# The layer norm's weight folded into the second matrix of the first MLP, on one core

## The reference, cut to what matters

```python
def _moe_ref(x, w_in, w_out, g_ln):          # x 2304 x 512, w_in 512 x 1024, w_out 1024 x 512
    h = x @ w_in
    h_max = np.max(h, axis=-1, keepdims=True)
    e = np.exp(h - h_max)
    sm = e / (np.sum(e, axis=-1, keepdims=True) + 1e-09)
    solu = h * sm
    mu = np.mean(solu, axis=-1, keepdims=True)
    var = np.mean((solu - mu) ** 2, axis=-1, keepdims=True)
    ln = (solu - mu) / np.sqrt(var + 1e-06) * g_ln
    return (ln @ w_out).astype(np.float32)
```

## Time and profile before

| | us |
|---|---|
| median of three runs | 934.86 (934.52 to 937.16) |
| the profiled execution, its own time | 934.9 |
| its span, first to last instruction | 933.2 |
| PE busy | 896.9 (96%) |
| DVE busy | 764.9 (82%) |
| ACT busy | 500.2 (54%) |
| POOL busy | 431.7 (46%) |

### The profile page before, as it was taken

The page is one execution under the profiler, slowest core; times in us unless marked ns, Lnnn a source line. Parts: engine busy times, 40 slices in busy tenths (PEclk is TensorE's granted clock), DMA queues, the critical chain, the costliest instruction groups (busy, mean ns, idle before and its releaser), DMA issues.

```text
span 933.2 us, 15150 instructions
## 1 busy us (share of the span) xinstructions
PE 896.9 (96%) x5416; PEld 740.5 (79%) x5416; DVE 764.9 (82%) x1306; ACT 500.2 (54%) x936; POOL 431.7 (46%) x445
## 2 busy tenths in 40 slices
PE   3899999999999999999999899999999999999997
PEld 1566666666667798998999788989999998989996
DVE  4889989899992948367362699999999999999997
ACT  2677777778773634334242555545545455545443
POOL 0443444444661833142140455656565556556563
PEclk9999999999999999999999999999999999999999
DMA  9234323403210100000000620000000000000000
GB/s 227 81 64 102 77 52 77 103 26 77 95 46 1 34 12 1 1 1 1 1 7 6 225 81 1 35 1 1 35 1 1 35 1 1 34 0 0 34 0 34
DMA packets 29026, 37.56 MB, mean 40 GB/s; under 512 B 3488, under 2 KB 16800, under 8 KB 28960
## 3 DMA queue, kind: packets, MB, share of 16 engines
q1 hardware_dynamic: 28240, 36.12, 14.0%
q10 hardware_dynamic: 720, 0.59, 0.3%
HBM read 31.98 MB, written 4.72 MB: 39 GB/s over the span
## 4 chain that ended last, share of the span: by engine, by line
DVE 49%; PE 44%; issue 4%; DMA 1%; ACT 1%; SPq 0%; POOL 0%; DVEq 0%
DVE g L835 13%; PE y_ps L1015 11%; PE s_ps L921 9%; PE o_ps L959 9%; PE t_ps L932 7%; DVE g_hi L839 7%; DVE g L825 7%; DVE g_lo L841 6%; PE h_ps L896 5%; DVE g L828 5%; DVE x_lo L691 2%; DVE solu L792 1%; DVE st_top L778 1%; DVE ln_lo L754 1%; DVE y_lo L767 1%
## 5 line engine op out<-in xcount | busy, mean ns | idle before, releaser
L433 POOL TENSOR_TENSOR w_lo<-w_raw,w_hi 128x512 fp32r<-128x512 f32 x96 | 131.8, 1373 | 161.3 <-ACT w_hi L613 161.3
L394 POOL TENSOR_SCALAR kept<-kept,inv 128x576 f32<-128x576 f32 x144 | 106.2, 755 | 155.6 <-DVE inv L728 155.6
L493 ACT ACTIVATE expd<-s_ps,ntop 128x576 f32<-128x576 f32 x144 | 104.8, 742 | 78.1 <-DVE ntop L696 78.1
L991 PE MATMUL m_ps<-y_hi,w_lo 128*128 128x384 f32 x384 | 130.9, 341 | 0.0
L991 PE MATMUL m_ps<-y_lo,w_hi 128*128 128x384 f32 x384 | 129.8, 338 | 0.0
L629 ACT ACTIVATE l<-u 128x384 f32<-128x384 f32 x96 | 50.6, 527 | 145.8 <-POOL u L441 145.8
L991 PE MATMUL m_ps<-y_hi,w_hi 128*128 128x384 f32 x384 | 128.5, 335 | 0.0
L441 POOL TENSOR_TENSOR u<-z,consts 128x384 f32<-128x384 f32 x96 | 105.9, 1103 | 41.9 <-ACT z L622 41.8
L696 DVE TENSOR_REDUCE ntop<-s_ps 128x1 f32<-128x576 f32 x144 | 106.1, 755 | 21.4 <-PE s_ps L921 15.1
L1072 PE MATMUL f_ps<-w_hi,g_hi 128*128 128x512 f32 x288 | 115.7, 402 | 8.1 <-DVE g_lo L841 8.1
L835 DVE TENSOR_TENSOR g<-g,l 128x384 f32<-128x384 f32 x96 | 119.1, 1240 | 2.8
(11 more groups left out here) (83 smaller groups left out, 1811.9 us busy)
## 6 DMA issues: line engine op xcount, KB each, us to landing
q_sb<-q_t SPq DMA_DIRECT2D x32, 288.0 KB, 5.2
v_sb<-v_main SPq DMA_DIRECT2D x16, 256.0 KB, 3.2
stage<-w_in SPq DMA_DIRECT2D x16, 256.0 KB, 2.7
w_raw<-w_out SPq DMA_DIRECT2D x8, 512.0 KB, 6.3
out<-o_sb SPq DMA_DIRECT2D x5, 768.0 KB, 3.5
k_sb<-k_t SPq DMA_DIRECT2D x21, 144.0 KB, 4.6
stage<-w_in SPq DMA_DIRECT2D x4, 512.0 KB, 10.1
stage<-w_out SPq DMA_DIRECT2D x4, 512.0 KB, 3.6
```

What stands on the lines that cost most here:

```text
L394: nc.gpsimd.tensor_scalar(kept[:, tile % RING, :], kept[:, tile % RING, :], inv[:, group % 2, k:k + 1], 1.0, ALU.mult, ALU.mult).then_inc( ...
L433: nc.gpsimd.tensor_tensor(w4[1][:, n % 2, :], w4_raw[:, n % F2, :], f32(w4[0][:, n % 2, :]), ALU.subtract).then_inc(w4lo_made, 1)
L991: last = nc.tensor.matmul(m_ps[n % 4][:, 0:GC], w[:, k, (n % F2) * P:(n % F2 + 1) * P], y[odd][:, k, :], start=(k == 0 and m == 0), stop=( ...
```

## The change

The weight g_ln is no longer multiplied into every row of ln. It is loaded with its 1024 values as a 128 x 8 tile (value k*128+p on partition p, column k), early on SP's queue. Since ln @ w_out sums over the hidden columns, the rows of w_out are scaled by it once: in `w_high` ScalarE multiplies each half (128 x 512) of a piece of w_out in place with an ACTIVATE whose scale is a column of that tile, waits for both, and then casts as before. This makes eight new instructions and four waits.

For each tile the product on VectorE (L807) goes. GpSimd makes ln = (solu + nmean) * rstd in one TENSOR_SCALAR with two pointer scalars in place of the TENSOR_TENSOR on ln (L421), straight from solu. The wait for the last transpose (lt_made) moves from VectorE to it. solu(t) on VectorE waits for ln(t-2), since GpSimd now reads the solu buffer. GpSimd's program of the first MLP is written out for all 18 tiles.

```diff
--- before.py
+++ after.py
@@ -99,6 +99,7 @@
         ident = sb("ident", [P, P])
         tau_sb = sb("tau_sb", [P, 1])
         consts = sb("consts", [P, 5])
+        gain = sb("gain", [P, F1])
 
         xt = sb("xt", [P, 2 * PG * C * GC])
 
@@ -139,12 +140,11 @@
         x_lo = sb("x_lo", [P, 2, C, P], FP32R, where=phase)
 
         ln = sb("ln", [P, 2, DFF1], where=phase)
-        gain = sb("gain", [P, DFF1], where=phase)
         e1 = sb("e1", [P, 2, DFF1], where=phase)
         solu = sb("solu", [P, 2, DFF1], where=phase)
         names = "top ntop esum esum_e inv ssum nmean sq msq var rstd"
         st = {n: sb("st_" + n, [P, 2], where=phase) for n in names.split()}
-        first_words = 2 * 2 * C * P + 7 * DFF1 + 2 * len(st)
+        first_words = 2 * 2 * C * P + 6 * DFF1 + 2 * len(st)
         sb("gap1", [P, SCORE_WORDS - first_words], where=phase)
         ln_hi = sb("ln_hi", [P, F1, GC], FP32R, where=phase)
         ln_lo = sb("ln_lo", [P, F1, GC], FP32R, where=phase)
@@ -212,7 +212,8 @@
         xhi_made, xlo_made = sem("xhi_made"), sem("xlo_made")
         h_made, htop_made, hntop_made = sem("h_made"), sem("htop_made"), sem("hntop_made")
         e1_made, ese_made, hinv_made = sem("e1_made"), sem("ese_made"), sem("hinv_made")
-        solu_made, mean_made, z_made = sem("solu_made"), sem("mean_made"), sem("z_made")
+        solu_made, mean_made = sem("solu_made"), sem("mean_made")
+        w2_scaled = sem("w2_scaled")
         sq_made, msq_made = sem("sq_made"), sem("msq_made")
         var_made, rstd_made = sem("var_made"), sem("rstd_made")
         ln_made, lt_made = sem("ln_made"), sem("lt_made")
@@ -324,6 +325,8 @@
                 load_values(pair)
             for n in range(STAGES):
                 sp.dma_start(staged(n)[0], staged_source(n)).then_inc(stage_in[n], 16)
+            sp.dma_start(gain[:, :], gain_d.rearrange("(k p) -> p k", p=P),
+                         allow_slow_non_contiguous=True).then_inc(gain_in, 16)
             for unit in range(2, UNITS):
 
                 sp.wait_ge(s_made, UNIT * (unit - 1))
@@ -334,7 +337,6 @@
                 for pair in (2 * unit, 2 * unit + 1):
                     load_values(pair)
 
-            sp.dma_start(gain[:, :], gain_d.partition_broadcast(P)).then_inc(gain_in, 16)
             for n in range(STAGES, W_ITEMS):
 
                 sp.wait_ge(w_lo, parts(n - STAGES + 1))
@@ -417,14 +419,17 @@
                 nc.gpsimd.tensor_tensor(st["rstd"][:, col], st["var"][:, col], consts[:, 0:1],
                                         ALU.pow).then_inc(rstd_made, 1)
                 pool.wait_ge(rstd_made, tile + 1)
-                pool.wait_ge(z_made, tile + 1)
-                nc.gpsimd.tensor_tensor(ln[:, slot, :], ln[:, slot, :],
-                                        st["rstd"][:, col].broadcast_to([P, DFF1]), ALU.mult).then_inc(ln_made, 1)
+                pool.wait_ge(mean_made, tile + 1)
+
+                wait(pool, lt_made, tile - 1)
+                nc.gpsimd.tensor_scalar(ln[:, slot, :], solu[:, slot, :], st["nmean"][:, col], st["rstd"][:, col],
+                                        ALU.add, ALU.mult).then_inc(ln_made, 1)
                 if isinstance(i, int) and i == 0 and n < 4:
 
                     w_low(C + n)
 
-            three_parts(pool, MT, 6, norm, MT // 6)
+            for tile in range(MT):
+                norm(tile // 6, tile % 6)
 
 
             def w4_low(j, n):
@@ -471,6 +476,14 @@
             def w_high(n):
                 src, hi, lo = staged(n)
                 act.wait_ge(stage_in[n % STAGES], 16 * (n // STAGES + 1))
+                if C <= n < C + F1 // 2:
+
+                    act.wait_ge(gain_in, 16)
+                    for a in range(2):
+                        m = 2 * (n - C) + a
+                        nc.scalar.activation(src[:, a, :], src[:, a, :], ACT.Copy, scale=gain[:, m:m + 1]
+                                             ).then_inc(w2_scaled, 1)
+                    act.wait_ge(w2_scaled, 2 * (n - C) + 2)
                 nc.scalar.copy(hi, src).then_inc(w_hi, 1)
 
             def w1_high(m):
@@ -789,6 +802,8 @@
                     dve.wait_ge(ese_made, tile + 1)
                     nc.vector.reciprocal(st["inv"][:, col], st["esum_e"][:, col]).then_inc(hinv_made, 1)
                     dve.wait_ge(hinv_made, tile + 1)
+
+                    wait(dve, ln_made, tile - 1)
                     nc.vector.scalar_tensor_tensor(out=solu[:, slot, :], in0=h_ps[slot][:, :],
                                                    scalar=st["inv"][:, col], in1=e1[:, slot, :],
                                                    op0=ALU.mult, op1=ALU.mult,
@@ -798,15 +813,6 @@
                                             ALU.mult).then_inc(mean_made, 1)
                 if not after_product(i, n):
                     transposed_low(i, n - 2)
-                if within(tile, MT):
-                    dve.wait_ge(mean_made, tile + 1)
-
-                    wait(dve, lt_made, tile - 1)
-                    if isinstance(tile, int) and tile == 0:
-                        dve.wait_ge(gain_in, 16)
-                    nc.vector.scalar_tensor_tensor(out=ln[:, slot, :], in0=solu[:, slot, :],
-                                                   scalar=st["nmean"][:, col], in1=gain[:, :],
-                                                   op0=ALU.add, op1=ALU.mult).then_inc(z_made, 1)
                 if isinstance(i, int) and tile == MT - 1:
 
                     for m in range(EARLY):
```

## The result

The changed kernel takes 940.4 us, the median of six runs (937.35 to 941.54), and the kernel before 934.68 us beside it. The ratio is 1.0053, with a 95% interval of [1.0035, 1.0072]: slower by half a per cent, where 938.4 us was forecast. The profiled execution took 940.83 us, its span 938.9 us against 933.2, so 5.7 us more.

A forecast was written before the change was run, and what follows sets the result against it. VectorE was taken to bound tiles 1 to 4 of the first MLP, PE afterwards. 934.9 us plus 4.7 for four longer tiles, less 1.2 for PE's stops, gave 938.4 us; range 932.7 to 941.2, the forecast's own 936.8 to 940.

The forecast's parts named there:

- one mechanism: First MLP, four tiles: w_lo starts before x_lo asks, x_lo waits for all of it; 938.4 us, chance 0.62.
- rival 3: First MLP: same mechanism but dearer, w_lo taking its whole 2.85 us, tile 8.9 us, sum 940.5 us; chance 0.10.
- GpSimd's new ln: GpSimd, each tile of the first MLP: TENSOR_SCALAR of 1024 columns with two pointers takes 1.2 us, upper bound 1.90.
- rival 1: First MLP: x_lo comes first if ln takes over 1.43 us; 6.94 us a tile, 932.7 us; chance 0.20.
- ScalarE's copies: ScalarE, w_out scaling in tiles 0 to 3: two copies at 0.62 us each, about 1.2 us a piece, four times.
- S: End of a tile's square on ScalarE, from which times are set; x_lo was forecast able to start at S+2.68.
- x_lo behind w_lo: First MLP, four tiles: w_lo starts at S+2.45, 0.23 us before x_lo asks; x_lo ends at S+5.29.
- The length of a tile: First MLP, tiles 0 to 3: 8.36 us each, so solu(4) starts 4.7 us later.
- The gain per group: First MLP after the first tiles: PE's stops of about 0.4 us once a group go, 1.2 us in all.
- The clock: PE at the first y: a long stop may drop the granted clock to 0.50, adding 1.5 us; part of rival 3.
- Rival 2: First MLP: copies lie in ScalarE's idle time, x_lo is free, all six PE stops go; 930.9 us, chance 0.08.
- VectorE's removed product: VectorE, first MLP: 18 times 1.28 us, 23 us of VectorE time; only PE's stops count, 1.2 us won.

The follow-up runs named there:

- experiment 9: Kernel before with only GpSimd's ln as a TENSOR_SCALAR and its program written out; VectorE's product kept, w_out unscaled: 929.54 us, again 930.34 us.
- experiment 1: Changed kernel with one more wait, so that GpSimd's w_lo starts only after x_lo of three tiles on: 933.54 us, 0.9984 of the kernel before.
- experiment 7: Changed kernel with one needless GpSimd instruction (128 x 512) ahead of ln in tiles 0 to 3: 933.48 us, 0.9984 of the kernel before.
- experiment 5: Changed kernel with GpSimd's w_lo of each piece of w_out as two instructions of 512 columns: 934.43 us, 0.9994 of the kernel before.
- the late load: Changed kernel with the weight's load moved back behind the last loads of attention: 938.69 us, 1.0049 of the kernel before.

## Why the prediction was right, point by point

The forecast was slower by 3.5 us by one mechanism, and the mechanism is shown. The measured difference is 5.7 us of the medians, the profiled one 5.9. The median of 940.4 lies 0.4 above the upper end that I gave my own forecast (936.8 to 940) and beside rival 3's 940.5, but w_lo did not take the 2.85 us of rival 3: it is my mechanism with the clock's fall on top.

- **GpSimd's new ln**: 1.2 us forecast from kept's row, 1.20 measured. This was the number on which forecast and rival 1 parted (1.43 us). That it is exact is luck. A row of the kernel before that I had not used is the same instruction as kept with two constants in place of the pointer, 0.07 us shorter than kept's 747 ns:

```profile
L401 POOL TENSOR_SCALAR k_sb<-k_sb x14: 672/676/681, 29.2 to 234.8; 128x576 f32<-128x576 f32 x14
```

With one pointer 576 columns take 0.747 us and 1024 take 1.13 (experiment 9), so 0.85 ns a column and not 0.98, and the second pointer adds 0.07 (1.13 to 1.20). My price a column was too high by about what the second pointer costs.
- **ScalarE's copies**: taken at 0.62 us each from the cast's row, measured 0.707. x_lo asked at S+2.86, not S+2.68. The trace thus sides with the Trainium skill (ScalarE: Activation LUTs, on what ACT_TABLE_LOAD costs), by which each pointer operand adds 93 ns: 0.707 is 0.09 above the cast. No run has this copy without its pointer. As said, it does not change the sum, only how clearly x_lo comes too late: by 0.43 us where 0.23 was forecast.
- **x_lo behind w_lo**: as forecast in each of four tiles; 2.55, 2.53, 2.50 and 2.41 us long. The "about 3 us" that I had named did not fit my own times, which give 2.6 (S+2.68 to S+5.29).
- **The length of a tile**: 8.36 forecast, 8.47 measured (33.86 / 4), mostly since w_lo alone takes 2.40 and not 2.3. Four tiles: 5.1 us more, not 4.7.
- **The gain per group**: 1.2 forecast, 1.9 measured. This term was mis-sized. I took PE's idle time (0.4 a stop) for the cost of a stop. From transpose 3 to transpose 15 the kernel with w_lo waiting (experiment 1), which has no stop there, takes 144.43 us (330.17 to 474.60) against 146.33: 0.63 for each of three stops. Transpose 15, before and in experiment 1:

```profile
476.41 1.03 PE L1026 MATMUL lt_ps<-ident,ln 128*128 128x128 f32 x8
...
474.60 1.03 PE L1033 MATMUL lt_ps<-ident,ln 128*128 128x128 f32 x8
```

The other 0.2 us is counted as busy: a matmul of h shows 0.39 us, but the next one starts 0.23 behind it where nothing waits, and the transposes behind a stop take 1.09 us instead of 1.03.
- **The clock**: named in rival 3 and given 1.5 us if it struck the first y, but left out of the sum. It struck in both profiles of the changed kernel and cost 1.6 us in the first. It is the greater part of what the forecast lacks. In the profiled execution the rest is 1.0 us from before solu(0), which is not of the change, and 0.4 in the tiles, against 0.7 more won in the groups. These partly cancel, so the sum came nearer than its terms.
- **Rival 1** (932.7 us) is what experiments 1 and 7 are, 933.5. **Rival 2** (930.9 us) is what the kernel does once the copies are out of the way, 930.1 to 930.7.

What I had not seen is that the gain did not need the change. I priced VectorE's removed product as the gain, though the same rows showed that x_lo's 2.24 us was mostly GpSimd's ln.

It stays open why the clock falls at the first y in some runs and not in others. With the late load PE's stops were 3.82 and 1.17 us, and the clock was back at 1.00 for the first y; with 3.82 and 1.85 it was not, twice. That is too few to say which stop does it.

## What to carry to other kernels

Where VectorE and GpSimd exclude each other, do not add up their work; look at which instruction of the one stands in front of which of the other, and how long that one is. A quicker instruction can let a longer one slip in front: a head start of 0.4 us made x_lo wait 1.8 us here, and the tile 1.4 us longer (8.5 against 7.1). So keep the long GpSimd instructions behind the VectorE ones that the chain needs, by a wait (experiment 1), or cut them up (experiment 5). One-time work such as scaling a weight belongs where its engine is idle, not where it first fits in the code. And try the cheaper form of an instruction on its own before a rewrite that contains it.

## What the runs showed of the hardware that was not expected

- The port goes over between two instructions. When an x_lo waited, it got in at the end of the GpSimd instruction in front, even though the next GpSimd one was ready (experiment 5: 1.45 us, then 1.75 for the second half).
- On GpSimd one ln of 128 x 1024 in fp32 takes 1.90 us as a TENSOR_TENSOR with a repeated column, 1.13 as a TENSOR_SCALAR with one pointer, and 1.20 with two; the TENSOR_TENSOR of two full tiles (w_lo) takes 2.40 when nothing of VectorE gets ahead of it, and 2.85 when an x_lo does.
- A stop of PE ahead of a transpose cost more than its idle time: 0.63 us for 0.4.
